# Dense experts 1 to 7 of a two-stage mixture of experts: the first layer as seven block products instead of eight, weights streamed in halves of an expert

## The reference

```python
out = np.zeros((N, D), dtype=np.float32)          # N, D, E, F = 1152, 512, 8, 1024
for e in range(E):
    h = np.maximum(x @ w1[e], 0.0)                # 1152x512 @ 512x1024
    ye = h @ w2[e]                                # 1152x1024 @ 1024x512
    out += P[:, e:e + 1] * ye
```

## Time and profile before

| | |
|---|---|
| median of 3 runs | 1253.88 us (1252.88 to 1254.04) |
| the profiled execution: its time | 1254.22 us |
| its span, first to last instruction | 1252.5 us |
| mean granted clock of PE | 0.994 of 2.4 GHz |
| PE busy | 1229.0 us (98%) |
| DVE, ACT, POOL busy | 485.8 us (39%), 364.9 us (29%), 154.6 us (12%) |
| stages, from the trace | attention to about 165 us, first mixture to about 430 us, dense expert 0 to 553.4 us, dense experts 1 to 7 to about 1250 us |

### The profile page before, as it was taken

How to read it: one execution, slowest core, us unless ns; L and a number is a source line. 1 busy time by engine, 2 the same in 40 slices (tenths; PEclk the granted TensorE clock), 3 DMA queues, 4 the chain that set the end, 5 groups by cost and what they waited for, 6 DMA issues and landing times.

```text
span 1252.5 us, 17819 instructions
## 1 busy us (share of the span) xinstructions
PE 1229.0 (98%) x6781; PEld 1096.1 (88%) x6781; DVE 485.8 (39%) x1089; ACT 364.9 (29%) x702; POOL 154.6 (12%) x235
## 2 busy tenths in 40 slices
PE   8999799999999899999999999999999999999998
PEld 5888688888888788999999999999999999999997
DVE  6555575544444532442133233233224214214321
ACT  5665244444444231131122122122122113112110
POOL 8767011111101430000000000000000000000000
PEclk9999989999999999999999999999999999999999
DMA  7760634444456530011011011002002101100000
GB/s 172 172 168 12 236 123 151 158 156 169 174 181 207 166 127 35 1 68 68 1 68 67 0 67 67 0 31 102 1 0 73 61 0 67 67 0 0 25 25 25
DMA packets 23970, 103.01 MB, mean 82 GB/s; under 512 B 4590, under 2 KB 9198, under 8 KB 19962
## 3 DMA queue, kind: packets, MB, share of 16 engines
q1 hardware_dynamic: 17498, 85.97, 20.7%
q0 software_dynamic: 3360, 11.01, 3.0%
q10 hardware_dynamic: 3072, 5.51, 1.3%
HBM read 87.74 MB, written 10.30 MB: 78 GB/s over the span
## 4 chain that ended last, share of the span: by engine, by line
PE 92%; DVE 3%; POOL 1%; DMA 1%; issue 1%; ACT 1%; POOLq 0%; DVEq 0%
PE bank L742 14%; PE bank L741 14%; PE bank L740 14%; PE bank L722 13%; PE bank L724 13%; PE bank L723 13%; PE bank L668 4%; PE bank L651 1%; PE bank L617 1%; PE bank L652 1%; PE bank L774 1%; DMA x_sb<-x_dram,gather_at 1%; POOL q_two L505 0%; PE bank L686 0%; PE bank L631 0%
## 5 line engine op out<-in xcount | busy, mean ns | idle before, releaser
L722 PE MATMUL bank<-xTh,w1h 128*128 128x384 f32 (+1 forms) x1024 | 342.7, 335 | 3.0 <-DVE xTl L1185 1.6
L723 PE MATMUL bank<-xTl,w1h 128*128 128x384 f32 (+1 forms) x1024 | 340.3, 332 | 0.0
L724 PE MATMUL bank<-xTh,w1l 128*128 128x384 f32 (+1 forms) x1024 | 340.2, 332 | 0.0
L989 ACT ACTIVATE hh<-bank 128x384 fp32r<-128x384 f32 (+1 forms) x256 | 123.4, 482 | 653.6 <-PE bank L724 650.9
L742 PE MATMUL bank<-w2h,hl 128*128 128x512 f32 (+1 forms) x768 | 302.8, 394 | 0.0
L741 PE MATMUL bank<-w2l,hh 128*128 128x512 f32 (+1 forms) x768 | 301.1, 392 | 0.0
L740 PE MATMUL bank<-w2h,hh 128*128 128x512 f32 (+1 forms) x768 | 300.6, 391 | 0.0
L1205 DVE SCALAR_TENSOR_TENSOR hl<-bank,hh 128x384 fp32r<-128x384 f32 (+1 forms) x256 | 139.3, 544 | 368.0 <-ACT hh L989 363.8
L722 PEld LDWEIGHTS bank<-xTh,w1h 128*128 128x128 f32 x1024 | 193.5, 189 | 5.3 <-issue 3.8
L723 PEld LDWEIGHTS bank<-xTl,w1h 128*128 128x128 f32 x1024 | 193.6, 189 | 1.2
L724 PEld LDWEIGHTS bank<-xTh,w1l 128*128 128x128 f32 x1024 | 193.3, 189 | 0.0
(11 more groups left out here) (173 smaller groups left out, 715.7 us busy)
## 6 DMA issues: line engine op xcount, KB each, us to landing
raw<-in_w SPq DMA_DIRECT2D x15, 2048.0 KB, 8.1
raw<-in_w1b SPq DMA_DIRECT2D x8, 2048.0 KB, 7.7
raw<-in_w2b SPq DMA_DIRECT2D x8, 2048.0 KB, 7.9
k_raw<-in_kT SPq DMA_DIRECT2D x16, 288.0 KB, 5.3
y_dram<-x_sb ACTq DMA_DIRECT2D x16, 256.0 KB
q_raw<-in_qT SPq DMA_DIRECT2D x8, 288.0 KB, 5.1
q_two<-w2l SPq DMA_DIRECT2D x8, 288.0 KB, 6.0
x_dram<-x_sb SPq DMA_DIRECT2D x1, 2304.0 KB, 9.3
```

The lines of the kernel that those rows point to most:

```text
L722: pe.matmul(dst, w1h[:, c, fs], xTh[:, c, ts], start=(c == 0), stop=False)
L723: pe.matmul(dst, w1h[:, c, fs], xTl[:, c, ts], start=False, stop=False)
L724: mm = pe.matmul(dst, w1l[:, c, fs], xTh[:, c, ts], start=False, stop=(c == DC - 1))
L989: act.activation(hh[:, f, 0:n_cols], bank[:, f % UP_BANKS, 0:n_cols], ACT.Relu).then_inc(st.hh_ready, 1)
```

## The change

Experts 1 to 7 of the dense stage are computed otherwise; everything up to the end of expert 0 keeps its arithmetic.

**First layer.** The 512 x 1024 weights of an expert are cut in halves along both sides, and so are the tokens (576 and 576). A block product of 2 x 2 by 2 x 2 blocks takes eight products of blocks. Strassen's scheme, in the variant with shared sums, takes seven: of the x blocks four sums T1 to T4 are formed once, of the weight blocks four sums S1 to S4 for each expert, and the seven products go to four PSUM banks. Two of the additions happen in PSUM (a second product onto the first), the others on DVE.

**Halves.** An expert runs in two halves of its hidden values, p = 0 and 1. A half takes 256 columns of each of the two sides of w1 (raw1_part, 1 MB, in runs of 1 KB), and the matching four chunks of w2 (raw2_part, 1 MB). `up_half` has four iterations (j, fi), each of seven products; a product is 2 chunks x 3 matmuls of 288 columns. `down_half` makes all nine tiles of tokens with four chunks each, 12 matmuls of 512 columns a tile, and DVE adds each tile to x_sb. An expert has 336 matmuls of 288 columns and 216 of 512.

**DVE, ACT, POOL.** In each iteration DVE forms five sums (z, v, c22, c12, c21) and four low parts, ACT copies the first product (p1_sum), takes four relus and rounds one chunk of w2, and POOL makes the low part of that chunk. Between `up_half` and the next one, during `down_half`, DVE forms S1 to S4 and seven low parts of 512 values, and ACT seven high parts.

**Setup.** While expert 0 runs, POOL adds xTh and xTl back together and forms T1 to T4 (eight operations of 1152 values), ACT rounds them, POOL makes their low parts (four more). In the last block of expert 0 the four ACT copies and four DVE subtractions of `split_w1(DN, 1)` give way to the first half's forms. PE now waits, before expert 1, for ACT's copy of the last tile (`DN.y_added`) and for DVE's last scaling, after which DVE raises `HV.h_ready`. SP loads the first half of w1 once the x forms are ready, and the first half of w2 once PE is through with expert 0.

The new buffers lie over old ones; the layout alone is left out below.

```diff
+        def product(to, form, x_of, j, fi, onto=False, mid=False):
+            dst = bank[:, to, 0:COLS]
+            fs = slice(fi * P, (fi + 1) * P)
+            for c in range(2):
+                xh, xl = x_of(c, j)
+                pe.matmul(dst, formh[:, form, c, fs], xh, start=(c == 0 and not onto), stop=False, skip_group_check=onto or mid)
+                pe.matmul(dst, formh[:, form, c, fs], xl, start=False, stop=False, skip_group_check=onto or mid)
+                mm = pe.matmul(dst, forml[:, form, c, fs], xh, start=False, stop=(c == 1), skip_group_check=onto or mid)
+            mm.then_inc(HV.product_done, 1)
+        def up_half(i, p):
+            for n, (j, fi) in enumerate(ITERATIONS):
...
+                first = (0, 4)[n % 2]
+                form_there(0)
+                pe.wait_ge(HV.h_ready, 4 * it + (4 * at + 2))
+                product(first, A11, of_x(0, 0), j, fi, mid=True)
+                form_there(1)
+                pe.wait_ge(HV.z_ready, it + (at + 1))
+                product(1, S2, of_form(T2), j, fi)
+                form_there(2)
+                pe.wait_ge(HV.c12_ready, it + (at + 1))
+                product(2, S1, of_form(T1), j, fi, mid=True)
+                form_there(3)
+                pe.wait_ge(HV.c21_ready, it + (at + 1))
+                product(3, S3, of_form(T3), j, fi, mid=True)
+                form_there(4)
+                pe.wait_ge(HV.p1_copied, it + (at + 1))
+                product(first, A12, of_x(1, 0), j, fi, onto=True)
+                form_there(5)
+                pe.wait_ge(HV.v_ready, it + (at + 1))
+                product(2, S4, of_x(1, 1), j, fi, onto=True)
+                form_there(6)
+                pe.wait_ge(HV.c22_ready, it + (at + 1))
+                product(3, A22, of_form(T4), j, fi, onto=True)
+        def down_half(i, p):
+            for n, t in enumerate(DOWN_ORDER):
+                pe.wait_ge(HV.y_added, 2 * NT * i + (NT * p + n + 1 + NT - Y_BANKS))
...
+                for l in range(FL):
+                    if n == 0:
+                        pe.wait_ge(HV.w2_ready, 2 * FL * i + (FL * p + l + 1))
+                    pe.matmul(dst, parth[:, l, ts], part2h[:, l, :], start=(l == 0), stop=False)
+                    pe.matmul(dst, parth[:, l, ts], part2l[:, l, :], start=False, stop=False)
+                    mm = pe.matmul(dst, partl[:, l, ts], part2h[:, l, :], start=False, stop=(l == FL - 1))
+                mm.then_inc(HV.down_done, 1)
+        pe.wait_ge(x_form_ready, 4)
+        pe.wait_ge(DN.h_ready, FC * NB + UP_BANKS)
+        pe.wait_ge(DN.y_added, NT + Y_BANKS)
...
+            def hidden_half(i, p):            # DVE
+                for n, (j, fi) in enumerate(ITERATIONS):
...
+                    v.wait_ge(HV.product_done, 7 * it + (7 * at + 2))
+                    v.wait_ge(HV.p1_copied, it + (at + 1))
+                    v.tensor_tensor(z_sum[:], banks[1], p1_sum[:], ALU.add).then_inc(HV.z_ready, 1)
...
+                    v.tensor_tensor(v_sum[:], banks[2], z_sum[:], ALU.add).then_inc(HV.v_ready, 1)
...
+                    v.tensor_tensor(sums[c22], banks[3], v_sum[:], ALU.add).then_inc(HV.c22_ready, 1)
+                    low_hidden(i, p, n, 0, c22, sums[c22])
+                    low_hidden(i, p, n, 1, c11, banks[0])
...
+                    v.tensor_tensor(sums[c12], banks[2], z_sum[:], ALU.add).then_inc(HV.c12_ready, 1)
...
+                    v.tensor_tensor(sums[c21], banks[3], z_sum[:], ALU.add).then_inc(HV.c21_ready, 1)
+                    low_hidden(i, p, n, 2, c12, sums[c12])
+                    low_hidden(i, p, n, 3, c21, sums[c21])
...
+            def far_half(i, p, follows):      # DVE
...
+                hidden_half(i, p)
...
+                for step in form_steps(i + p, 1 - p) if follows else ():
+                    if step in (1, 3, 5):
+                        added(i, p, n)
+                        n += 1
+                for n in range(n, NT):
+                    added(i, p, n)
...
+            def hidden_half(i, p):            # ACT
+                for n, (j, fi) in enumerate(ITERATIONS):
...
+                    act.copy(p1_sum[:], bank[:, (0, 4)[n % 2], 0:COLS]).then_inc(HV.p1_copied, 1)
+                    act.wait_ge(HV.c22_ready, it + (at + 1))
+                    act.activation(parth[block_of(1, 1, fi, j)], sums[block_of(1, 1, fi, j)], ACT.Relu).then_inc(HV.hh_ready, 1)
...
+                    if n == 0:
+                        act.wait_ge(HV.raw2_loaded, 32 * i + (16 * p + 16))
+                        act.wait_ge(HV.down_done, 2 * NT * i + (NT * p + NT))
+                    act.copy(part2h[:, n, :], raw2_part[:].rearrange("p s l d -> p (s l) d")[:, n, :]).then_inc(HV.w2h_ready, 1)
...
-                    split_w1(DN, 1)
-            dense(DN, 1)
```

More of the change, by code:

```diff
@@ L589, in _, with whole, less @@
                 pool.tensor_tensor(w2l[:, f, :], raw2[:, f, :], w2h[:, f, :].bitcast(F32), ALU.subtract).then_inc(DN.w2_ready, 1)
+            def whole(k, b):
+                c, n = slice(2 * k, 2 * k + 2), slice(b * TOKENS, (b + 1) * TOKENS)
+                pool.tensor_tensor(quarters[:, 2 * k + b], xTh[:, c, n].bitcast(F32), xTl[:, c, n].bitcast(F32), ALU.add).then_inc(x_form_sums, 1)
+            def less(to, a, b, after):
+                pool.wait_ge(x_form_sums, after)
+                pool.tensor_tensor(quarters[:, to], quarters[:, a], quarters[:, b], ALU.subtract).then_inc(x_form_sums, 1)
+            pool.wait_ge(DN.xTl_ready, NT + XT_BANKS)
+            whole(0, 0)
+            whole(0, 1)
+            less(0, 1, 0, 2)
+            whole(1, 1)
+            less(1, 3, 1, 4)
+            less(3, 3, 0, 5)
+            whole(1, 0)
+            less(2, 2, 3, 7)
+            for n, form in enumerate((T1, T3, T2, T4)):
+                pool.wait_ge(x_formh_ready, n + 1)
+                pool.tensor_tensor(x_form_l[form], quarters[:, X_FORM_AT[form]], x_form_h[form].bitcast(F32), ALU.subtract).then_inc(x_form_ready, 1)
+            with pool.Fori(0, E - 1) as i:
+                for p in range(2):
+                    for l in range(FL):
+                        pool.wait_ge(HV.w2h_ready, 2 * FL * i + (FL * p + l + 1))
+                        pool.tensor_tensor(part2l[:, l, :], raw2_part[:].rearrange("p s l d -> p (s l) d")[:, l, :],
+                                           part2h[:, l, :].bitcast(F32), ALU.subtract).then_inc(HV.w2_ready, 1)
         @block.tensor
@@ L890, in _ @@
+            pe.wait_ge(x_form_ready, 4)
+            pe.wait_ge(DN.h_ready, FC * NB + UP_BANKS)
+            pe.wait_ge(DN.y_added, NT + Y_BANKS)
+            with pe.Fori(0, E - 1) as i:
+                for p in range(2):
+                    up_half(i, p)
+                    down_half(i, p)
         @block.scalar
@@ L1069, in after_step, with high_x_form, high_forms @@
                     act.activation(share[:, 1], g, ACT.Exp, bias=one_row[:, 3:4]).then_inc(softplus, 1)
+            def high_x_form(form):
+                n = (T1, T3, T2, T4).index(form)
+                act.wait_ge(x_form_sums, X_FORM_SUMS[n])
+                act.copy(x_form_h[form], quarters[:, X_FORM_AT[form]]).then_inc(x_formh_ready, 1)
+            def high_forms(i, p):
+                act.wait_ge(HV.raw1_loaded, 32 * i + (16 * p + 16))
+                for form in FORM_ORDER:
+                    block = {A11: (0, 0), A12: (0, 1), A22: (1, 1)}.get(form)
+                    if block is None:
+                        act.wait_ge(HV.form_summed, 8 * i + (4 * p + {S1: 1, S3: 2, S2: 3, S4: 4}[form]))
+                    act.copy(formh[:, form], forms[:, form] if block is None else raw_block(*block)).then_inc(HV.formh_ready, 1)
             for b in range(NB):
@@ L1217, in dense_expert @@
                 v.wait_ge(st.y_added, NT * e + Y_BANKS)
[L1218 removed]
+                v.tensor_copy(share_now[:, m, :], share[:, m, :, bass.ds(e, 1)].rearrange("p t a -> p (t a)")).then_inc(over_share_taken, 1)
                 for b in range(NB):
@@ L1438 @@
+            with v.Fori(0, E - 2) as i:
+                for p in range(2):
+                    far_half(i, p, True)
+            far_half(E - 2, 0, True)
+            far_half(E - 2, 1, False)
 GATES_SPLIT = 3 + 6
```

268 lines of the change are left out of this document (226 added, 42 removed).

## The result

| | before | changed |
|---|---|---|
| median of the runs | 1253.95 us | 1220.57 us |
| ratio, 95% interval | | 0.9731 (0.9714 to 0.9748) |
| the same kernel again, another session | 1253.53 us | 1219.18 us, 0.9725 (0.9707 to 0.9743) |
| profiled execution shown here | 1254.22 us | 1216.94 us |

The forecast was 1226 us, with 1217 to 1243 as the range. The first profile of the changed kernel was taken in a slower execution, with a lower granted clock in the attention (0.88, against 0.99 in the profile of before), so its rows are taken from the second session's profile, at about the clock of before (0.995 and 0.994 on average). Between these two the difference is 37.3 us; the medians differ by 33.4 us (34.4 in the second session). So the forecast of -28.4 us missed by 5.4 us by the medians, and by 8.9 us at equal clock; that the medians come nearer is luck.

The account below looks back on a forecast made before the run. PE was taken as the bound, its matmuls following one another through experts 1 to 7. First layer -29.8 us plus entry 1.4 us gave -28.4 us, so 1226 us against 1254.2; range 1217 to 1243.

Parts of the forecast that it names:

- What bounds the kernel: Experts 1 to 7: PE bounds, the stage lasting as long as its matmuls at 173.4 and 228.9 ns, 695.8 us.
- The first layer: Experts 1 to 7: 2352 matmuls at 136 ns, 319.9 us, 29.8 us less; bounds 131.8 ns (512/384 line) to 140 ns.
- The weight load: First-layer matmuls: loads overlap and could follow at about 103 ns, under the 120 ns that 288 columns take.
- The second layer: Down parts of experts 1 to 7: 216 matmuls of 512 columns an expert at 228.9 ns, no change.
- DVE and ACT: Iterations of up_half: DVE busy 4.1 of 5.7 us, ACT 2.6, least spare 1.0 us, so PE never waits.
- rival A: Product chain in up_half: spare missing, PE waits each iteration; 0.3 us each is 17 us, 1243 us; chance 13%.
- POOL beside DVE: Setup during expert 0: POOL's work does not slow DVE's, from one overlapping operation of 0.79 against 0.75 us.
- The entry: Before expert 1: PE waits for ACT's last copy and DVE's last scaling, starting 1.4 us late, once.
- DMA and forms: Loads and weight forms between halves: hidden; forms ready 11.1 us into a 24.7 us down part, 13.6 us early.
- B: First-layer matmuls: a floor in the distance, 150 ns giving 1258.7 us, deciding from 148.1 ns; chance 6%.
- C: First-layer matmuls: the weight load does not overlap at all, 222.5 ns, 1429 us; chance under 1%.
- D: First-layer matmuls: the extra beside the columns vanishes, about 122.5 ns, 1194 us; chance 2%.

Follow-up runs that it names:

- experiment 10: Kernel before, first-layer matmuls of experts 1 to 7 cut to 288, 320, 336 and 352 columns: 133.3, 146.7, 155.8 and 160.8 ns from start to start.
- experiments 5 to 7: Changed kernel with three, six and one more DVE operations of 288 values ahead of z in each iteration: 1232.65, 1305.54 and 1216.34 us.
- experiment 8: Changed kernel with one more POOL subtraction of 512 values, both operands in SBUF, after each low part of w2: 1224.21 us.
- experiments 3 and 4: Changed kernel with DVE's first semaphores raised before its last three scalings, 1216.82 us; the same with no w2 rounding in a half's first iteration, two in the second, 1216.18 us.

## Why the prediction was right

- **What bounds the kernel.** Right. The stage is the sum of its two distances, before and after, to within 0.5 us.
- **The first layer.** The mechanism was right, the size was off. The step was "For 288 columns (120.0 ns) I take 16 ns, as in the two nearest widths: 136 ns". It measured 12.4 ns (132.4), 2352 x 3.6 ns = 8.5 us too dear, and that is all but 0.4 us of the error of 8.9 at equal clock. By the medians the forecast was 5.4 us off, because the median of the changed kernel lies 3.6 us above the profile; that is luck. Both its profiles have the same 659.0 us in the stage. The nearest widths were a poor guide: 336 is dearer by its width (experiment 10), and the 320 was one pair in the attention, 150 ns, where a row of 24 has 146.7. The 384, with most rows and the same kind of stream, had 13.4 and would have given 133.4 ns, 6 us nearer. The lower bound, 131.8, held.
- **The weight load.** Right that it does not bind at 288: the floor is about 112 ns. The two sentences of the Trainium skill's page "TensorE: Matmul & The Clock Gate" that I set against the rows fail as the rows said. By "Back-to-back issue gap", columns over 2.4 GHz plus 2.5 ns would be an estimated 122.5 ns, and 132.4 was measured. By "What overlaps and what doesn't", a load would not overlap here; but loads are shown with 0.19 us each, longer than the distance of 132.4 ns, so they are hidden.
- **The second layer.** Right: 228.9 ns.
- **DVE and ACT.** Right that PE never waits for them, and nearly right in their prices (ACT's relus of sums take 446 ns, not 403). The statement under rival A that "from 0.51 us each the gain is gone" was never reached. But the spare was read as the time by which a result is early, 1.0 us (0.9 measured). The room of a chain that comes round every iteration is what its engine has left in a round, 0.7 to 0.8 us by the cycle (experiments 5 to 7). The conclusion stood; the margin was smaller than said.
- **POOL beside DVE.** The step "If POOL's work slowed DVE's ... so nothing" was wrong as a reading. One overlap of 0.24 us between a long and a medium operation was taken to show that there is no exclusion. There is one: the longest low part takes 1.55 us instead of 0.46 (experiment 8). In the changed kernel it adds (532 - 459) x 168 = 12 us to DVE's busy time and nothing to the total. It could have been seen before: five operations of L1355 start during one of POOL's subtractions (L589) there, not one, and all end 0.55 us after it and take 784 to 792 ns, where the four others take 743 to 752.
- **The entry.** 1.4 us forecast, 1.4 measured from start to start (1.25 of them shown as idle time). The first half of w2 was put at 0 to 1 us, none taken: ACT waits 0.7 us for it and PE does not notice. It shows as soon as the gap is closed (experiments 3 and 4).
- **DMA and forms.** Forms were forecast ready 11.1 us into the down part; the last one ends 10.2 us in. A transfer of 1 MB takes 6.1 us to land, more than half of the 7.7 us of 2 MB; it is hidden as forecast.
- **Rivals.** B needed a floor from 148.1 ns on: refuted by 132.4 at 288 columns and 112 at 192. C (222.5) and D (122.5) are refuted by the 132.4 too. A is not there at nine operations and is at twelve.

## What to carry to other kernels

Where PE is the bound, price a change by number of matmuls times the start-to-start distance at the new width, measured over a row of them in the same kind of stream, and ask of every width by itself: a split that cuts an eighth of the work can hand back a seventh of its gain in narrower matmuls (6.2 of 44.5 us here). For an engine that must keep up, compare its whole round, waits on others included, with that of the bound; how early one result comes says only how large a single delay may be. And place GpSimd operations with SBUF inputs beside VectorE operations that read PSUM, not beside those that read SBUF twice: here the first kept 0.45 us and the second ended 0.3 us after POOL whenever they began.

## What the runs showed of the hardware that was not expected

A matmul of 128 rows by 128 weights in float32r, each with its own weight load, followed the last after about 112 ns and no less at either width tried below 288: 111.9 at 192 columns, 112.4 at 240. Above that the distance is the columns at 2.4 GHz plus 12 to 16 ns, and the extra depends on the width: 12.4 at 288 in the new stage (13.3 in the old one), 13.3 at 320, 15.8 at 336, 14.2 at 352, 13.4 at 384, 15.6 at 512. It is not the width alone: in the run with 240 columns the same matmuls of 512 had 20.0. A VectorE operation with both operands in SBUF that starts during a GpSimd operation with both operands in SBUF ends 0.31 to 0.32 us after it (288 values, all 168 cases of two traces); with one operand in PSUM it takes 0.45 us all the same. DVE operations of 288 values are shown with 450 ns, but start 0.37 us apart when nothing is waited for, so that busy time overstates what a further one costs.
